# Attention and two feed-forward layers on one core: the first two heads' score operands made by halves, and the first five groups of tiles in another order

## What is computed

```python
q_bits = (q @ proj > 0)            # 6 bits a position, and the same of k
mask = q_bucket[:, :, :, None] == k_bucket[:, :, None, :]
scores = where(mask, (q @ k.T) / sqrt(64), -1e9)
attn = exp(scores - max(scores));  attn /= sum(attn) + 1e-9
x = attn @ v                       # 1536 x 512 once the heads are side by side
h = maximum(maximum(x @ w1, x @ w2), x @ w3);  y = h @ w_out
g = (y @ w_in2) * sigmoid(1.702 * y @ w_in2);  out = g @ w_out2
```

## Time and profile before

| | |
|---|---|
| median of 3 runs | 666.23 us (665.66 to 666.4) |
| profiled execution | 665.83 us, of which the span is 664.0 us |
| PE busy | 656.9 us, 99% of the span |
| DVE, POOL, ACT busy | 505.7, 474.0, 346.5 us |
| granted TensorE clock | full in all 40 slices |

### The profile page before, as it was taken

How to read it: one execution, slowest core, us unless ns; L and a number is a source line. 1 busy time by engine, 2 the same in 40 slices (tenths; PEclk the granted TensorE clock), 3 DMA queues, 4 the chain that set the end, 5 groups by cost and what they waited for, 6 DMA issues and landing times.

```text
span 664.0 us, 11816 instructions
## 1 busy us (share of the span) xinstructions
PE 656.9 (99%) x3820; PEld 568.7 (86%) x3820; DVE 505.7 (76%) x988; ACT 346.5 (52%) x749; POOL 474.0 (71%) x538
## 2 busy tenths in 40 slices
PE   8999999999999999999999999999999999999998
PEld 6776777777677799999999999988889889898896
DVE  6889889898887898879698863778877665555554
ACT  6887887877877530110104353555555554544433
POOL 6774765888876999878852347999977777777710
PEclk9999999999999999999999999999999999999999
DMA  6976847847460111011110201212222133222102
GB/s 144 163 153 142 170 110 150 159 96 166 113 179 7 34 33 33 33 33 43 38 47 1 96 1 60 69 48 79 92 69 64 65 121 102 64 65 67 46 16 96
DMA packets 77309, 54.17 MB, mean 82 GB/s; under 512 B 47457, under 2 KB 66305, under 8 KB 77249
## 3 DMA queue, kind: packets, MB, share of 16 engines
q1 hardware_dynamic: 75600, 53.02, 32.2%
q10 hardware_dynamic: 1648, 0.39, 0.3%
HBM read 32.51 MB, written 3.15 MB: 54 GB/s over the span
## 4 chain that ended last, share of the span: by engine, by line
PE 82%; POOL 9%; issue 3%; DVE 3%; ACT 1%; DVEq 0%; POOLq 0%; ACTq 0%
PE psR L1655 8%; PE psO L1572 8%; PE psR L1656 7%; PE psR L1654 7%; PE psR L1558 7%; PE psS L1550 6%; PE psS L1654 6%; PE psS L1655 6%; PE psS L1656 6%; PE psS L1757 4%; PE psS L1756 4%; PE psS L1755 4%; POOL w_lo L750 2%; POOL probs L591 2%; POOL early L640 1%
## 5 line engine op out<-in xcount | busy, mean ns | idle before, releaser
L591 POOL TENSOR_SCALAR probs<-probs,lone,inv 128x768 f32<-128x768 f32 x96 | 94.0, 986 | 52.1 <-DVE inv L1168 52.0
L750 POOL TENSOR_TENSOR w_lo<-w_raw,w_hi 128x256 fp32r<-128x256 f32 x96 | 78.5, 832 | 43.3 <-ACT w_hi L999 42.5
L819 ACT ACTIVATE probs<-psS,neg_max 128x768 f32<-128x768 f32 x96 | 86.5, 901 | 21.6 <-DVE neg_max L1151 20.3
L1151 DVE TENSOR_REDUCE neg_max<-psS 128x1 f32<-128x768 f32 x96 | 91.1, 950 | 8.0 <-PE psS L1550 7.7
L1558 PEld LDWEIGHTS psR<-ident,probs 128*128 128x128 f32 x576 | 65.8, 140 | 24.2 <-POOL probs L591 15.6
L574 POOL TENSOR_SCALAR w_hi<-w_raw 128x256 fp32r<-128x256 f32 (+1 forms) x79 | 48.6, 618 | 51.4 <-PE psS L1656 30.1
L1558 PE MATMUL psR<-ident,probs 128*128 128x128 f32 x576 | 81.5, 276 | 0.7 <-POOL probs L591 0.2
L828 ACT ACTIVATE probs_t<-psR 128x384 f32<-128x384 f32 x131 | 62.6, 489 | 21.0 <-PE psR L1558 20.1
L1572 PE MATMUL psO<-probs_t,v_raw 128*64 128x384 f32 x384 | 68.8, 494 | 0.0
L1407 DVE TENSOR_TENSOR v_raw<-psR,early 128x384 f32<-128x384 f32 x64 | 35.3, 552 | 33.1 <-PE psR L1656 32.8
L1412 DVE TENSOR_TENSOR v_raw<-v_raw,bits 128x384 f32<-128x384 f32 x64 | 52.4, 821 | 5.6 <-ACT bits L1022 2.9
(11 more groups left out here) (277 smaller groups left out, 1878.8 us busy)
## 6 DMA issues: line engine op xcount, KB each, us to landing
w_raw<-in_moe_w_in SPq DMA_DIRECT2D x16, 512.0 KB, 3.4
w_raw<-in_moe_w_out SPq DMA_DIRECT2D x32, 256.0 KB, 2.8
w_raw<-in_moe_w SPq DMA_DIRECT2D x9, 512.0 KB, 3.8
h_lo<-w_hi SPq DMA_DIRECT2D x22, 192.0 KB, 3.5
h_hi<-w_hi SPq DMA_DIRECT2D x18, 192.0 KB, 3.3
v_raw<-in_v SPq DMA_DIRECT2D x16, 192.0 KB, 2.5
stacks<-w_hi SPq DMA_DIRECT2D x16, 192.0 KB, 3.8
out<-results SPq DMA_DIRECT2D x11, 256.0 KB, 2.2
```

The source lines that it names most:

```text
L591: pool.tensor_scalar(probs[i % PROBS][:, :], probs[i % PROBS][:, :], lone[:, i % 6:i % 6 + 1], inv[:, i % 6:i % 6 + 1], ALU.add, ALU.mult) ...
L750: pool.tensor_tensor(in2_slot(w_lo, n, which), in2_raw(n, PARTS2[which]), f32(in2_slot(w_hi, n, which)), ALU.subtract).then_inc(in2_split, 1)
L819: act.activation(probs[i % PROBS][:, :].rearrange("p (a b) -> p a b", a=2), psS[i % 2][:, :, 0:HALF], ACT.Exp, bias=neg_max[:, i % 6:i % 6 ...
L1151: dve.tensor_reduce(neg_max[:, i % 6:i % 6 + 1], psS[i % 2][:, :, 0:HALF], AX.XY, ALU.min).then_inc(max_ready, 1)
```

## The change

The stacks of heads 0 and 1 are made in halves of 384 queries, and each half has its own wait. Tables say which engine makes which part, as (part, head, half), half 2 being both. DVE's half differences, `scalar_tensor_tensor` included, go partly to POOL. The order of calls changes on PE, ACT, DVE and POOL up to and with group 4, and the loops begin at group 5. On SP only the wait ahead of L502 changes. The diff, cut:

```diff
+    ACT_PARTS = (("q_hi", 0, 0), ("q_marks", 0, 0), ("k_marks", 0, 0), ("q_marks", 0, 1), ("q_hot", 1, 0),
+                 ("k_marks", 1, 1), ("k_marks", 1, 0), ("q_marks", 1, 1))
+    DVE_PARTS = (("q_hi", 0, 1), ("k_hi", 0, 2), ("k_lo", 0, 1), ("k_lo", 0, 0), ("k_hi", 1, 2), ("q_hot", 0, 0),
+                 ("q_marks", 1, 0))
+    GPS_PARTS = (("k_hot", 0, 2), ("q_lo", 0, 0), ("q_hi", 1, 0), ("k_marks", 0, 1), ("q_lo", 0, 1),
+                        ("k_lo", 1, 1), ("k_lo", 1, 0), ("q_hot", 0, 1), ("q_lo", 1, 0), ("q_hi", 1, 1),
+                        ("q_lo", 1, 1), ("q_hot", 1, 1))
...
+        def stacked_by(sem_, table, wanted):
+            done = [n + 1 for n, part in enumerate(table) if part in wanted]
+            return [(sem_, max(done))] if done else []
...
+        def first_done(a, j):
+            return (act_first, 1 if a == 0 else 2 + j) if (a, j) != (0, 1) else (dve_first, 1)
...
-            sync.wait_ge(act_stacked, 4)
+            for part_done in stacked(("k_hi", 1, 2)):
+                sync.wait_ge(*part_done)
             sync.dma_start(f32(stack(1, K_HOT)[0:D, :]), f32(stack(1, K_LO)[D:P, :])).then_inc(first_placed, 16)
...
+            def alone(part):
+                if GPS_PARTS.index(part) > 0:
+                    pool.wait_ge(pool_stacked, GPS_PARTS.index(part))
+
...
+            def first_q_lo(a, j):
+                alone(("q_lo", a, j))
+                for part_done in stacked(("q_hi", a, j)):
+                    pool.wait_ge(*part_done)
+                pool.tensor_tensor(half(stack(a, Q_LO)[D:P, :], j), half(qk_t[a][0:D, :], j),
+                                   f32(half(stack(a, Q_LO)[0:D, :], j)), ALU.subtract).then_inc(pool_stacked, 1)
...
+            first_k_hot(0)
+            first_q_lo(0, 0)
+            first_q_hi(1, 0)
+            first_k_marks(0, 1)
+            first_q_lo(0, 1)
+            first_k_lo(1, 1)
+            first_k_lo(1, 0)
+            first_q_hot(0, 1)
+            first_q_lo(1, 0)
+            pool.wait_ge(pool_stacked, 9)
+            norm(0)
+            first_q_hi(1, 1)
+            norm(1)
+            pool.wait_ge(probs_normed, 2)
+            first_q_lo(1, 1)
+            pool.wait_ge(pool_stacked, 11)
+            make_qk_hi(2)
+            first_q_hot(1, 1)
+            norm(2)
+            norm(3)
+            make_qk_lo(2)
+            norm(4)
+            norm(5)
+            make_qk_hi(3)
...
             exp_tile(4)
             copy_qk(3, 0)
+            copy_qk(3, 1)
             exp_tile(5)
-            copy_qk(3, 1)
-            copy_turned(1, 1)
             copy_turned(2, 0)
...
+            first_copy_qk(0, 1)
+            first_q_hi(0, 1)
+            first_k_hi(0)
+            first_k_lo(0, 1)
             dve.wait_ge(marks_made, 10)
             make_first_bits(0)
...
+            first_k_lo(0, 0)
+            first_k_hi(1)
+            first_q_hot(0, 0)
             make_first_bits(1)
             row_max(0)
+            first_q_marks(1, 0)
             row_max(1)
             invert_sums(0, 1)
...
             row_max(3)
+            copy_turned(0, 0)
+            row_max(4)
             invert_sums(2, 1)
-            row_max(4)
             row_max(5)
             invert_sums(3, 2)
...
             scores(0)
+            turn_qk(2)
             scores(1)
-            turn_qk(2)
             scores(2)
...
             turn_probs(1, 0)
+            turn_probs(1, 1)
             scores(5)
             turn_qk(3)
-            turn_probs(1, 1)
             scores(6)
             turn_probs(2, 0)
+            turn_probs(2, 1)
             scores(7)
-            turn_probs(2, 1)
             turn_probs(3, 0)
             turn_probs(3, 1)
             scores(8)
             project(1)
+            scores(9)
             turn_probs(4, 0)
             turn_probs(4, 1)
-            scores(9)
...
+            scores(12)
+            turn_probs(9, 0)
+            turn_probs(9, 1)
+            turn_probs(10, 0)
+            scores(13)
+            for c in range(TH, NT):
+                times_values(0, c)
+            scores(14)
+            turn_probs(10, 1)
+            turn_probs(11, 0)
+            turn_probs(11, 1)
-            for n in range(4, GROUPS + 1):
+            for n in range(5, GROUPS + 1):
```

More of the change, by code:

```diff
@@ new lines, in first_q_hi @@
+            def first_q_hi(a, j):
+                alone(("q_hi", a, j))
+                pool.wait_ge(*first_done(a, j))
+                copy(half(stack(a, Q_LO)[0:D, :], j), half(qk_t[a][0:D, :], j)).then_inc(pool_stacked, 1)
+            def first_q_lo(a, j):
[4 more added lines that the diff above has]
+                                   f32(half(stack(a, Q_LO)[0:D, :], j)), ALU.subtract).then_inc(pool_stacked, 1)
@@ new lines, in first_q_hot, with first_k_lo @@
+            def first_q_hot(a, j):
+                alone(("q_hot", a, j))
+                pool.wait_ge(*first_done(a, j))
+                copy(half(stack(a, Q_HOT)[0:D, :], j), half(qk_t[a][0:D, :], j)).then_inc(pool_stacked, 1)
+            def first_k_lo(a, j):
+                alone(("k_lo", a, j))
+                pool.wait_ge(*first_done(a, j))
+                for part_done in stacked(("k_hi", a, 2)):
+                    pool.wait_ge(*part_done)
+                pool.tensor_tensor(half(stack(a, K_LO)[0:D, :], j), half(qk_t[a][D:P, :], j),
+                                   f32(half(stack(a, K_LO)[D:P, :], j)), ALU.subtract).then_inc(pool_stacked, 1)
@@ new lines, in first_k_hot, with first_k_marks @@
+            def first_k_hot(a):
+                alone(("k_hot", a, 2))
+                for j in range(2):
+                    pool.wait_ge(*first_done(a, j))
+                copy(stack(a, K_HOT)[0:D, :], qk_t[a][D:P, :]).then_inc(pool_stacked, 1)
+            def first_k_marks(a, j):
+                alone(("k_marks", a, j))
+                pool.wait_ge(*emptied(("bits", 0, a)))
+                copy(half(stack(a, K_HOT)[D:D + MARKS, :], j),
+                     f32(first_marked[a][32 * (2 + j):32 * (2 + j) + MARKS, :])).then_inc(pool_stacked, 1)
@@ L659, in _ @@
                 pool.wait_ge(proj_signed, n + 1)
[L660 to L670, removed]
@@ new lines, in _ @@
+            first_q_hot(1, 1)
[5 more added lines that the diff above has]
+            make_qk_hi(3)
+            norm(6)
+            norm(7)
+            norm(8)
+            make_qk_lo(3)
+            norm(9)
+            norm(10)
+            norm(11)
+            norm(12)
+            norm(13)
+            make_qk_hi(4)
+            make_qk_lo(4)
+            for n in range(5, GROUPS + 1):
+                p, st = n // 4, n % 4
+                norm(3 * n - 1)
@@ L1546, in scores @@
                 for which, (qs, ks, rows) in enumerate(((Q_LO, K_LO, P), (Q_HOT, K_HOT, D + MARKS))):
+                    if n < 2 and t % TH == 0 and which == 1:
+                        for part_done in stacked(("q_hot", a, t // TH), ("q_marks", a, t // TH), ("k_hot", a, 2), ("k_marks", a, 0),
+                                                 ("k_marks", a, 1)):
+                            pe.wait_ge(*part_done)
+                        if a == 1:
+                            pe.wait_ge(first_placed, 16)
                     if n >= 2 and t == 0 and which == 1:
```

176 lines of the change are left out of this document (95 added, 81 removed).

## The result

The changed kernel takes 667.69 us (median of 9 runs, 667.13 to 668.3), against 665.70 for the kernel before in the same sets: a ratio of 1.0027, 95% interval 1.0019 to 1.0036, so 2.0 us slower. The forecast was 667.7. The profiled execution took 667.18, 1.35 over the one of before. The two traces tell where that comes from, and not all of it is where the forecast put it.

What follows compares the result with a forecast made beforehand. PE's fixed work bounds the kernel, with SP's placings 0.2 us from binding: tile 15 +2.04 less 0.53 gives +1.5 on the profiled 665.83, 667.3, and 0.4 for the median gives 667.7; eight in ten 665.2 to 669.0.

Steps and rivals of the forecast that it cites:

- SP's chain: SP's fixed DMA order from place_lo(2), begun at 24.75, to place_lo(3), issued at 39.0 and landed at 42.2 for tile 15.
- rival B: SP issues at its undisturbed pace, 13.3 us, landing at 40.8 to 41.2; net +0.1 to +0.5, 666.5; chance 0.17.
- What is given back behind tile 15: From tile 15 to tile 18, the 0.53 us lost over PE's pace before the change would be regained in full.
- PE's side: PE's reordered work up to tile 15 alone: tile 15 at 40.0, 0.13 earlier, with 0.6 to 0.7 us gained in all.
- the 1 to 3 that were to show the forecast right: Sign: PE idle 1 to 3 us ahead of tile 15, up to 1.7 within tile 12, released by head 3's DMA.
- The hand count: Recorded durations carried through the new order: tile 10 at 28.1, first product with the values at 29.6 against 29.73.
- Splitting its wait gains nothing: 0: Tile 0 still starts at 10.60; its latest part, a POOL marks copy at 10.5 to 10.9, is wanted at 11.0.
- POOL's list up to tile 3: POOL's copies and half differences, 7.95 us plus 0.4 to 1.0 for DVE's disturbance, end at 15.7; tile 3 at 15.8.
- C: Rival: PE's order pays and place_lo(3) lands by 40.0, needing make_qk_lo(2) by about 23.5; 665.2; chance 0.15.
- D: Rival: late halves of head 1 and norms cost PE 0.7 ahead of tile 10, marks stall adds; +3.2, 669.4; chance 0.05.
- the late placing: The forecast's main case: SP's late placing of head 3 stalls tile 15, 2.04 us later; 667.7; chance 0.63.

Runs made afterwards that it cites:

- before_norm3: The kernel before with norm(3) ahead of make_qk_lo(2) on POOL and nothing else; ratio 1.0012, 0.75 us over before.
- after_q5: The kernel after with load_qk(5) issued by SP ahead of place_lo(2); 666.97 us, ratio 1.0017 to before.
- after_cols: The kernel after with only invert_sums' two-column DVE operations made a column at a time; 666.38 us.
- after_hot: The kernel after with head 0's Q_HOT copy of the first half made by ACT instead of DVE; 667.83 us, ratio 1.0032 to before.
- best2: The kernel after with Q_HOT copy on ACT, column-wise DVE operations, load_qk(5) issued by ACT, place_lo(3) ahead of place_marks(3) on SP; 670.96 us.

## Why the prediction was right, and where it was not

**The time** was right: 667.7 forecast, 667.69 measured, and tile 15 at 42.2 forecast, 42.02 measured. That close a match is partly luck. The change was forecast at +1.5 us on the profiled execution, which measured +1.35, and 0.4 was added because the median of three runs of before, 666.23, lay that much above its profile. Nine runs of before have their median at 665.70, below the profile. So by the medians the change costs 2.0, half a microsecond more than forecast, and the starting value that was too high by as much hides it. The parts cancel as well.

**SP's chain: right.** Start of `place_lo(2)` forecast 24.75, measured 25.20: the reciprocal of tiles 3 and 4 came 0.5 later than the bound taken from before, because tile 4 was late. From there to the second issue of `place_lo(3)`: forecast 14.25, measured 13.5, the undisturbed pace, as rival B had it. Landing 3.2 as forecast. The two misses, 0.45 later and 0.75 shorter, cancel to 0.3 us. That the chain binds is shown by before_norm3, by after_q5, and by the waits for the DMA of 0.32 to 1.57 in seven of the kernels, the one after among them.

**What is given back behind tile 15: right.** Forecast 0.53; counted from tile 0 the change adds 2.15 at tile 15 and 1.61 at tile 18. The prediction gave two reasons, the new order and the others catching up while PE waits. Each does it alone: after_q5 has the order and no wait, before_norm3 the wait and the old order, and both go from tile 15 to tile 18 in 6.3 us, where before takes 6.85.

**PE's side: wrong, and this is the step that failed.** "On PE's side alone tile 15 would start at 40.0, 0.13 earlier." (40.0 is 0.16 ahead of 40.16; the slip changes nothing.) It would start at about 41.4: after_q5, where SP is out of the way, has it 1.53 later than before, counted from tile 0. So PE stood 0.32 us ahead of tile 15, not the 1 to 3 that were to show the forecast right, and not at all inside tile 12. The hand count held up to tile 10 (28.37, 28.1 forecast), with tile 0 starting 0.3 earlier than it took; the first product with the values then came at 30.52, 29.6 forecast. Two terms were missing.
- Tile 0. "Splitting its wait gains nothing: 0" named a POOL part as its latest. That one ended at 10.01, in time. The latest was DVE's copy of Q_HOT at 11.52, for which the prediction has no term. It took 1.04 beside POOL. I had put a price on POOL being slowed by DVE, not on DVE being slowed by POOL. With SP's chain eased, this term is worth 0.37 at tile 18 and 0.58 in the median.
- Turn 6 and turn 8. The hand count took every `invert_sums` at its usual length. The collisions of two-column operations with `make_qk_hi(3)` and `make_qk_lo(3)` cost 1.0 us between tiles 10 and 12 (after_cols). The trace of before had one of 1.75, beside POOL's `make_qk_lo(3)`, in a place where PE did not wait. I had passed it over:

```profile
30.42 1.82 POOL L587 TENSOR_TENSOR w_lo<-w_raw,w_hi 128x768 fp32r<-128x768 f32 x1
```

```profile
30.52 1.75 DVE L1159 TENSOR_SCALAR lone<-neg_max 128x2 f32<-128x2 f32 x1
```

**POOL's list up to tile 3: half right.** Its end was forecast at 15.7, measured 15.14. Tile 3 started at 15.96, near the 15.8 forecast but by another cause: PE went to it without a wait, straight from the filler matmuls behind tile 2, and tile 2 had waited 0.82 for the exponential of the late tile 0.

**Rivals.** B had the right pace of SP and a wrong end, since it took SP's start as forecast and PE's side as free. C fell: `make_qk_lo(2)` ended at 25.17, not by 23.5, and PE's order did not pay. D named the effect of a late PE side (0.7 lost ahead of tile 10), not its cause, and priced it as if it would add; it lay beside SP's chain and was mostly hidden. Without the late placing the change would still be a loss of about 1.0 to 1.4 us (after_q5), which no case of the forecast held.

## What to carry to other kernels

A queue without a wait in its trace can still be the next bound. Add up what is in order behind the call that you move, and compare the landing with the time at which the consumer gets there; here 0.2 us of slack hid a chain of 19 us. Two chains of nearly the same length hide each other's losses: mending one may show nothing (after_hot) or a part (after_q5), and only mending both shows the sum. And look in the profile for instructions whose length varies for one shape: their long cases say who locks whom, and a new order may put such a case where somebody waits.

## What had not been expected of the hardware

- A DVE operation on 128x2 numbers in SBUF took 0.15 us or as much as 2.04, ending with POOL's instruction; the same on 128x1 took 0.156 at most, in 96 cases. The Trainium skill (SBUF — State Buffer, Who interferes with whom) tells of one pair of ports that DVE in its two-port mode and GpSimd hold for a whole instruction, the other fully blocked. The traces agree that one of the two stands for the whole of the other's instruction, and show it with two numbers to a partition; which ports were used they can't show. Splitting such an operation frees it, and made the kernel of before 0.37 us faster.
- DMA landings of 192 KB went from 3.0 to 7.3 us in best2, where a load in short runs was issued beside them from a second queue and another 192 KB placing stood right ahead of them.
- After PE had been busy for 1.85 of the 4 us from 40 to 44 in best2, its granted clock was 0.50 from 44 to 50 us, and full again from 51 on.
- Single DMA issues on SP were 1 us longer than their like, not in the same place in each execution (3.56 and 3.39 against 2.46 for `place_hi(3)`), which can shift the whole result by up to that much wherever SP binds. That fits the wider spread of the kernel after (667.13 to 668.3).
